# Writing out the attention's batch loops on four engines of a routed attention and MoE kernel

## The reference

```python
# 1. chunked attention: q, k, v (4, 8, 768, 64), 8 memory rows for each head
for c in range(24):                       # chunks of 32 queries
    q_c, k_ctx = q[:, :, 32*c:32*c+32], k[:, :, l_start:r_end]   # 16 to the left, 8 to the right
    k_full = concat(mem_k, k_ctx); v_full = concat(mem_v, v_ctx)
    out[:, :, chunk] = softmax(q_c @ k_full.T / 8) @ v_full
# 2. MoE with exact routing: 3072 tokens of 512, 8 experts of 1024, 384 tokens for each
#    (token, expert) pairs are taken in falling order of x @ w_gate, until an expert is full
out[mask] = relu(x[mask] @ w1[e]) @ w2[e]
# 3. dense layer: h = x @ w_in; u = h * softmax(h); out = layernorm(u) * g_ln @ w_out
```

## Time and profile before

| | before |
|---|---|
| median of 3 runs | 861.91 us |
| profiled execution | 860.36 us, of it the span 858.6 us |
| PE busy in the span | 84% |
| DVE, ACT, POOL busy | 64%, 37%, 39% |
| PE, in the chain that ended last | 60% |
| "issue", in that chain | 11% |
| mean DMA rate | 104 GB/s |

### The profile page before, as it was taken

The page is one execution under the profiler, slowest core; times in us unless marked ns, Lnnn a source line. Parts: engine busy times, 40 slices in busy tenths (PEclk is TensorE's granted clock), DMA queues, the critical chain, the costliest instruction groups (busy, mean ns, idle before and its releaser), DMA issues.

```text
span 858.6 us, 18982 instructions
## 1 busy us (share of the span) xinstructions
PE 719.1 (84%) x6837; PEld 620.4 (72%) x6838; DVE 550.8 (64%) x2135; ACT 317.9 (37%) x521; POOL 335.8 (39%) x243
## 2 busy tenths in 40 slices
PE   4768858311998999999998999999899989989993
PEld 3546646201896989789887988797898879888982
DVE  3434634686878677877787696878787876823140
ACT  2223424002314631462355146414623551473160
POOL 5790000007524740672175147406712750573001
PEclk9787978655899999999999999999999999999997
DMA  8987963005103311330132033113202320331000
GB/s 346 355 301 256 368 221 123 15 0 176 57 1 111 99 50 50 99 98 25 61 111 74 25 105 116 49 49 99 98 25 65 107 74 25 110 112 48 1 13 37
DMA packets 24935, 89.16 MB, mean 104 GB/s; under 512 B 3360, under 2 KB 3360, under 8 KB 24864
## 3 DMA queue, kind: packets, MB, share of 16 engines
q0 software_dynamic: 14208, 50.34, 17.8%
q1 hardware_dynamic: 10656, 37.97, 12.4%
HBM read 75.71 MB, written 12.58 MB: 103 GB/s over the span
## 4 chain that ended last, share of the span: by engine, by line
PE 60%; DVE 11%; issue 11%; POOL 8%; DMA 6%; ACT 2%; DVEq 0%; ACTq 0%; POOLq 0%; SPq 0%
PE bank L503 16%; PE bank L504 14%; PE bank L505 14%; POOL wl L1292 6%; DMA raw<-w,w_idx 4%; PE bank L436 3%; PE bank L393 2%; PE banks L418 2%; PE bank L403 2%; DMA unit<-unit_in 2%; PE bank L429 2%; DVE hits L958 1%; DVE hot_b L1039 1%; DVE z L1087 1%; PE banks L532 1%
## 5 line engine op out<-in xcount | busy, mean ns | idle before, releaser
L1286 POOL DMA_INDIRECT raw<-w,w_idx x60 | 59.4, 990 | 286.9 <-DVE w_idx L1007 249.6
L1292 POOL TENSOR_TENSOR wl<-raw,wh 128x1024 fp32r<-128x1024 f32 x60 | 155.7, 2595 | 26.1 <-ACT wh L729 24.8
L729 ACT ACTIVATE wh<-raw 128x1024 fp32r<-128x1024 f32 x60 | 63.4, 1056 | 92.7 <-DMA raw<-w,w_idx 92.6
L503 PE MATMUL bank<-xh,wh 128*128 128x384 f32 x256 | 91.3, 357 | 3.7 <-DVE xl L1133 3.4
L503 PE MATMUL bank<-hh,wh 128*128 128x384 f32 x256 | 90.1, 352 | 0.0
L505 PE MATMUL bank<-xh,wl 128*128 128x384 f32 x256 | 86.9, 340 | 0.0
L504 PE MATMUL bank<-xl,wh 128*128 128x384 f32 x256 | 86.9, 340 | 0.0
L505 PE MATMUL bank<-hh,wl 128*128 128x384 f32 x256 | 86.0, 336 | 0.0
L504 PE MATMUL bank<-hl,wh 128*128 128x384 f32 x256 | 85.9, 336 | 0.0
L503 PE MATMUL bank<-wout_h,uh 128*128 128x512 f32 x192 | 80.2, 417 | 0.0
L503 PE MATMUL bank<-win_h,yh 128*128 128x512 f32 x192 | 77.3, 402 | 0.0
(11 more groups left out here) (178 smaller groups left out, 1613.7 us busy)
## 6 DMA issues: line engine op xcount, KB each, us to landing
unit<-unit_in SPq DMA_DIRECT2D x24, 768.0 KB, 6.5
unit<-unit_in SPq DMA_DIRECT2D x24, 520.0 KB, 5.6
x_rows<-x_sb SPq DMA_DIRECT2D x24, 256.0 KB, 4.7
raw<-w_in POOLq DMA_DIRECT2D x4, 512.0 KB, 8.5
raw<-w_out POOLq DMA_DIRECT2D x4, 512.0 KB, 6.2
raw<-w,w_idx POOLq DMA_INDIRECT x60, 4.2
gath<-x_rows,ids POOLq DMA_INDIRECT x24, 3.7
out<-z,ids_prev POOLq DMA_INDIRECT x14
```

Source lines behind the costliest of these rows:

```text
L503: nc.tensor.matmul(bank, stat_h, mov_h, start=first, stop=False)
L729: nc.scalar.activation(wh[:, c % WCH, :], stage(s, c), ACT.Copy).then_inc(w_hi, 1)
L1286: gp.indirect_dma_start(stage(s, c), None, table, bass.IndirectOffsetOnAxis(ap=w_idx[:, c % WCH:c % WCH + 1], axis=0))\
L1292: gp.tensor_tensor(wl[:, c % WCH, :], stage(s, c), wh[:, c % WCH, :].bitcast(F32), ALU.subtract)\
```

## The change

The loop over `b` becomes a Python loop on the four engines, so that all 24 steps stand in the instruction streams one after the other. `b` is then a number: register arithmetic, compares and branches go, and waits compare with constants. Three functions look at whether their index is a number (`isinstance(u, int)`) to leave out waits of the first units; for units from 6 on no such condition holds, so waits and order stay as they are. The work of each step, its tiles, and the loop over the experts stay.

```diff
                 store(u, u)
-            with sp.Fori(0, B - 1) as b:
+            for b in range(0, B - 1):
                 for r in range(TPB):
                     load_qk(b * TPB + (r + 6), r)
                     load_v(b * TPB + (r + 5), r + 5)
...
                 step(i, i, i // 3 + 1, (i - 1) // 3 + 1)
-            with pe.Fori(1, B) as b:
+            for b in range(1, B):
                 for r in range(TPB):
                     step(b * TPB + r, r, b * 2 + (r // 3 + 1), b * 2 + ((r - 1) // 3 + 1))
...
             for i in range(TPB):
                 step(i, i)
-            with act.Fori(1, B) as b:
+            for b in range(1, B):
                 for r in range(TPB):
                     step(b * TPB + r, r)
...
                     normalise(i - 1, i - 1, None if i - 1 < 3 else 1)
-            with ve.Fori(1, B) as b:
+            for b in range(1, B):
                 for r in range(TPB):
                     soften(b * TPB + r, r, b * 2 + (1 if r == 0 else 2))
                     q = (r - 1) % TPB
```

## The result

The change makes the kernel slower by about half a per cent: median 866.28 us of 20 runs against 862.39 us of 20 runs of the kernel before, ratio 1.0046 with a 95% interval of 1.0024 to 1.0067. The execution profiled takes 865.45 us, of which the span is 863.7.

A forecast was written before the change was run, and what follows sets the result against it. TensorE's instruction fetch was taken to bound the attention: 12 packets at 5.54 us plus 9.07 give 75.5 against 67.95 us, so 860.36 + 7.6 = 868.0, given as 868.5 us, range 861.5 to 875 for 8 in 10.

The forecast's parts named there:

- TensorE executes faster than its instructions arrive: Attention: 125 matmuls run in 3.44 us, but an instruction packet for them comes only each 5.54 us.
- In the second pass the packet behind the loop's end was fetched over the loop's first one: TensorE's attention loop: code lost this way, so the next jump costs 7.50 us and the third pass stalls.
- The rival that went the other way: Attention: straight code is prefetched, the 7.50 us jump goes, the second pass keeps 23.76 us; 852.9 us, chance 0.07.
- The sum of +7.6: TensorE, stall ending at 79.50 to the last pass's end: 14 packets take 75.5 us in place of 67.95.
- The twelve packets: Packets of the changed attention fetched while unit loads run: 12 at 5.54 us, 66.5 us together.
- The two other packets: Last two packets of the attention, after the unit loads have ended: 9.07 us for both.
- The packet's own range: Time of one instruction packet in the attention: 5.2 to 6.0 us, giving +3.5 to +13.1 us, 864 to 873.5.
- the second stretch: The 864 matmuls of the former second loop pass: stalls each 125 matmuls, 34 to 40 us; wrong if under 29.
- The transposes: Transposes of the logits, behind the attention: to start at 162 us and not at 154.46.
- ScalarE, VectorE and SyncE: Other engines in the attention: removed branches and register arithmetic, longer streams and sooner load issue all taken as 0.
- TensorE's constants: Constants in place of registers: at most two instructions less for each of 18 steps, below 1 us, taken as 0.
- The third rival: Attention: loads get in front of each packet, 6.36 us for each, so 877.8 us; chance 0.08.

The follow-up runs named there:

- pad182: Kernel before, all loops kept, with 182 instructions added on TensorE ahead of step 0, under its wait for the first load: 846.31 us, ratio 0.9801.
- pad194: Kernel before, all loops kept, with 194 instructions added on TensorE ahead of step 0: 845.47 us, ratio 0.9794.
- others_only: Kernel before with the batch loops of SyncE, ScalarE and VectorE written out, TensorE keeping its loop: 860.83 us, ratio 0.9977.
- pad182_rest: pad182 with the loops of SyncE, ScalarE and VectorE also written out, TensorE's loop kept: 845.05 us, ratio 0.981 to the kernel before.
- after_light: Changed kernel, loading only q and a quarter of the value windows from the fourth unit on: 847.06 us, ratio 0.9826 to the kernel before.
- pe_only: Kernel before with only TensorE's loop over the batches written out, the other three engines keeping theirs: 870.61 us, ratio 1.0086.

## Why the prediction was right, point by point

- "TensorE executes faster than its instructions arrive" is shown. Stalls come each 125 matmuls where code is fetched (some too short to be listed), and none where it is held (pad182, pad194).
- "In the second pass the packet behind the loop's end was fetched over the loop's first one" is borne out by moving the loop in three ways, with the three outcomes that were foretold. The fetch itself is in no row; it is inferred from where the stalls come and from the count of packets.
- The rival that went the other way, 852.9 us with prefetched straight code, had 0.07. It is right for the jump, whose 7.5 us were all won, and wrong for the stream, where 15.7 us were lost in the second pass. The same branch costs 0.49 us when its target is still held and 7.50 when it is not. The Trainium skill (Runtime: NRT & Kernel Launch, Instruction fetch mechanics) says that branching breaks sequential prefetch and that kernels prefer full unrolling. The trace agrees on the jump of 7.50 us and not on the unrolling, which made the kernel slower by 0.5%.
- The sum of +7.6 stands against +4.84 in the profile. The twelve packets were set at 5.54 and took 5.36 each (64.27 for the 66.5 of the forecast), -2.2. The steps ahead of the sum's start, taken as unchanged, ended about 0.95 us sooner (the 1.44 of step 12 less the first jump's 0.49, which the sum had taken off already). The two other packets took some 0.4 us more than the 9.07 set for them. The first matmul's start, at 6.15 in place of 6.51, is not part of it: by the stall that ends at 24.20, for 24.21 before, this lead was gone. That packets simply vary is the likeliest reason for the rest, with 39.44 us for six steps and 33.82 for the next six, but the loads of units end within the second six, so that their share is not told apart.
- The packet's own range, 5.2 to 6.0, held, in its lower third. That the median of 866.28 lies only 2.2 us below the forecast's 868.5 is in part luck: the sum started from an execution of 860.36 us, 2.0 below the median of 20 runs of the kernel before. Median against median the change costs 3.9 us, about half of the 7.6.
- Of the signs named, the second stretch was to take 34 to 40 us and took 39.44, some 5 packets more were to come and 5 did, and the expert part was to be unchanged and took 704.4 us against 704.1. The transposes were to start at 162 and started at 159.3, by the terms above.
- ScalarE, VectorE and SyncE were set at 0. This is not contradicted: others_only and pad182_rest show no effect clear of noise. For TensorE's constants the prediction names 36 instructions, which is a seventh of a packet of 256 and not a sixth; the term stays below 1 us.
- The third rival, slower by more as data get in front, had a point in that the loads raise the price of a packet (after_light), but its 6.36 us was too high: 5.36 was measured.

## What to carry to other kernels

A loop written out is not free on an engine whose instructions are short: count the instructions, and compare the time in which the engine runs through a packet of them (here 3.44 us) with the time in which a packet arrives (here 5.4 us under load, 4.4 with light traffic). A loop that is held beats straight code there, if it and the packet ahead fit (8 packets here); look in the trace whether the first matmul after each jump has an "issue" stall of microseconds, and if so, move the loop's start by instructions laid under an existing wait, and read what they cost in the passes before. Wandering "issue" stalls at equal counts of matmuls are the sign to look for.

## What the runs showed beside it

The time of one kernel varies by 1.5% (856.86 to 869.61 us in 17 runs of the kernel before), and the profiles show one source of it outside the attention. The expert loop's passes are not all alike. These are the last five of the six looped experts in the kernel before, and in pe_only, whose TensorE code there is the same:

```profile
355.20:747.90 392.70, 372.36 (x2097) 1.00 0.23 74
```
```profile
356.70:759.00 402.30, 381.11 (x2097) 0.97 0.23 72
```

The same 2097 matmuls take 9.6 us more at a mean granted clock of 0.97: read in steps of 2 us, it stands at 0.50 for a short time, which is 1.2 GHz in place of 2.4, twice in the first of these passes and once in each other, and never in the kernel before. In the changed kernel both kinds of pass are in one execution, 79.70 us at 0.98 and 78.70 at 1.00:

```profile
357.80:437.50 79.70, 76.06 (x421) 0.98 0.22 73
...
596.00:674.70 78.70, 74.54 (x422) 1.00 0.23 74
```

Such a fall, and the wait ahead of it, in the first of the two:

```profile
364.88 0.20 PE L480 MATMUL bank<-cnt,same_expert 96*96 96x3 bf16 x1 [2.03 <-DVE hot_a L958]
```
```profile
367.00:369.00 2.00, 2.00 (x8) 0.50 0.30 37
```

In each pass TensorE stands twice for some 2 us, waiting for VectorE, and the clock falls after one of these waits in some passes and not in others. In pe_only the wait at L480 is 2.31 to 2.44 us long in all five passes, and the clock falls at or behind each; in the kernel before it is 1.48 to 2.10, and it never falls; in the changed kernel it falls after 2.03 and not after 2.09. What decides it was not tried. It accounts for the profile of pe_only, which is longer than that of the full change although its attention ended 1.9 us sooner: 402.30 against 395.20 us in the looped experts. That its median lies 4 us higher for the same reason is likely, but only one execution was profiled. For a change of half a per cent the profile of the stage that was changed is therefore a check that the medians need.
